# A one-core attention, expert-routing and feed-forward kernel: another order of the last attention steps, of expert 0's weight loads and of two weight splits

## The reference

```python
# 1 attention: batch 2, 8 heads, 768 rows, head size 64
k_sum = k.reshape(B, H, 24, 32, D).max(axis=3);  v_sum = v.reshape(B, H, 24, 32, D).mean(axis=3)
scores_l = q @ k^T / 8, kept where |i - j| < 16;  scores_s = q @ k_sum^T / 8 + log(32)
a = softmax(concat(scores_l, scores_s));  attn = a @ concat(v, v_sum)
# 2 experts: x is attn as 1536 rows of 512; 8 experts of 512 x 1024 x 512
logits = normalized(x) @ normalized(expert_emb).T / tau;  e = argmax(logits)
out[row] = softmax(logits)[e] * (relu(x[row] @ w1[e]) @ w2[e])
# 3 feed-forward, 512 x 2048 x 512
h = relu(out @ w_in);  result = h * h @ w_out
```

## Time and profile before

| | |
|---|---|
| median of 3 runs | 553.11 us (553.05 to 554.74) |
| profiled execution | 553.05 us, span 551.3 us, mean granted PE clock 0.986 |
| busy share of the span | PE 95%, DVE 49%, ACT 43%, POOL 16% |
| attention steps on PE, start to next start | `turn_probs` 0.8 us, `scores` 1.05, `values` 0.85, `fill` 0.6, `turn_pair` 0.8, `ranks` 1.0, `slots` 0.8 |
| steps on DVE | `scale_out` 0.7 us, `row_max` 0.8, `lay_blocks` 2.4, `place` 1.5, `make_hots` 1.6 |
| steps on ACT | `exps` 1.6 us, `regroup_q` 0.7, `move_k` and `move_q` 1.0, `move_prob` 0.45 for one head |

### The profile page before, as it was taken

The page is one execution under the profiler, slowest core; times in us unless marked ns, Lnnn a source line. Parts: engine busy times, 40 slices in busy tenths (PEclk is TensorE's granted clock), DMA queues, the critical chain, the costliest instruction groups (busy, mean ns, idle before and its releaser), DMA issues.

```text
span 551.3 us, 10956 instructions
## 1 busy us (share of the span) xinstructions
PE 523.8 (95%) x4442; PEld 473.1 (86%) x4442; DVE 269.4 (49%) x442; ACT 234.9 (43%) x413; POOL 89.0 (16%) x123
## 2 busy tenths in 40 slices
PE   7498977899999999999999999999999999999997
PEld 6387866789998989989889899899989989989995
DVE  6477877768485864757462232232223223232321
ACT  5478855655676653555531231222223123122221
POOL 5761111212543131260100000000000000000000
PEclk9789999899999999999999999999999999999999
DMA  7956678895679958768110020020001002001001
GB/s 215 257 154 176 186 182 251 251 338 176 251 260 331 312 160 275 263 229 275 64 47 1 0 77 1 1 76 0 0 21 56 0 0 76 0 0 38 2 2 38
DMA packets 62655, 69.50 MB, mean 126 GB/s; under 512 B 22512, under 2 KB 47088, under 8 KB 62232
## 3 DMA queue, kind: packets, MB, share of 16 engines
q1 hardware_dynamic: 59160, 57.36, 32.9%
q0 software_dynamic: 3456, 11.60, 6.2%
HBM read 58.88 MB, written 10.06 MB: 125 GB/s over the span
## 4 chain that ended last, share of the span: by engine, by line
PE 84%; SPq 5%; DVE 4%; DMA 4%; issue 1%; ACT 1%; POOL 0%; DVEq 0%; ACTq 0%; POOLq 0%
PE psum L917 26%; PE psum L918 25%; PE psum L919 25%; DMA k_raw<-in_k 2%; SPq L364 2%; PE psum L911 1%; PE psum L765 1%; PE psum L703 1%; DMA x_rows_sb<-x_rows,gather_tab 1%; SPq L366 1%; PE psum L1021 1%; SPq L363 1%; DVE wb_lo L1627 1%; DVE neg_max L1351 1%; PE psum L830 1%
## 5 line engine op out<-in xcount | busy, mean ns | idle before, releaser
L919 PE MATMUL psum<-x_hi,win_lo 128*128 128x256 f32 x384 | 108.7, 283 | 0.0
L918 PE MATMUL psum<-x_lo,win_hi 128*128 128x256 f32 x384 | 108.7, 283 | 0.0
L917 PE MATMUL psum<-x_hi,win_hi 128*128 128x256 f32 x384 | 108.5, 282 | 0.0
L1725 DVE TENSOR_TENSOR h_sq<-h_relu 128x512 f32<-128x512 f32 x48 | 33.2, 692 | 126.6 <-ACT h_relu L1291 126.6
L1291 ACT ACTIVATE h_relu<-psum 128x512 f32<-128x512 f32 x48 | 28.7, 597 | 127.4 <-PE psum L919 127.4
L917 PE MATMUL psum<-wb_hi,h_hi 128*128 128x512 f32 x208 | 82.4, 396 | 0.0
L919 PE MATMUL psum<-wb_hi,h_lo 128*128 128x512 f32 x208 | 81.1, 390 | 0.0
L918 PE MATMUL psum<-wb_lo,h_hi 128*128 128x512 f32 x208 | 81.1, 390 | 0.0
L918 PEld LDWEIGHTS psum<-x_lo,win_hi 128*128 128x128 f32 x384 | 73.6, 192 | 1.4
L917 PEld LDWEIGHTS psum<-x_hi,win_hi 128*128 128x128 f32 x384 | 73.6, 192 | 1.4
L919 PEld LDWEIGHTS psum<-x_hi,win_lo 128*128 128x128 f32 x384 | 73.6, 192 | 0.0
(11 more groups left out here) (211 smaller groups left out, 878.2 us busy)
## 6 DMA issues: line engine op xcount, KB each, us to landing
w_raw<-in_moe_w SPq DMA_DIRECT2D x56, 512.0 KB, 4.0
win_raw<-in_moe_w_in POOLq DMA_DIRECT2D x8, 512.0 KB, 8.1
w_raw<-in_moe_w_out SPq DMA_DIRECT2D x8, 512.0 KB, 3.6
k_raw<-in_k SPq DMA_DIRECT2D x8, 384.0 KB, 3.6
q_raw<-in_q SPq DMA_DIRECT2D x8, 384.0 KB, 5.5
v_blk<-in_v SPq DMA_DIRECT2D x3, 1024.0 KB, 8.0
v_win<-in_v SPq DMA_DIRECT2D x16, 192.0 KB, 3.9
x_rows<-x_all SPq DMA_DIRECT2D x8, 384.0 KB, 5.4
```

The lines of the kernel that those rows point to most:

```text
L917: pe.matmul(o, l_hi, r_hi, start=start, stop=False)
L918: pe.matmul(o, l_hi, r_lo, start=False, stop=False)
L919: return pe.matmul(o, l_lo, r_hi, start=False, stop=stop)
L1725: dve.tensor_tensor(h_sq[c % 2][:, :], h_relu[c % 2][:, :], h_relu[c % 2][:, :], ALU.mult)\
```

## The change

SP loads all eight parts of block 0 in one go and stores pairs 6 and 7 behind them. POOL loads and splits pieces 6 and 7 of w_in ahead of its loop. On PE, DVE and ACT the steps of the last three attention half-pairs and of batch 0's routing stand in another order. ACT moves more of the turned probabilities and of the turned pairs, in place of DVE, and `values(3, 1, 1)` stands ahead of `turn_rows(0)`.

```diff
@@ SP @@
                 for c in range(2 * PIECES):
-                    if first and c == PIECES:
-                        store_x(PAIRS - 2)
-                        sp.wait_ge(gathered, 32)
                     if not first:
                         sp.wait_ge(w_split[c], b)
...
             load_expert(0, blk_tab0, first=True)
-            store_x(PAIRS - 1)
+            for pr in range(PAIRS - 2, PAIRS):
+                store_x(pr)
@@ POOL @@
             scatter(2, scatter_tab0)
-            with pool.Fori(EARLY, nblk - 2) as b:
-                gather(b + 2, gather_tab)
-                scatter(b, scatter_tab)
             load_win(6)
             load_win(7)
             split_win(6, 3)
             split_win(7, 4)
+            with pool.Fori(EARLY, nblk - 2) as b:
+                gather(b + 2, gather_tab)
+                scatter(b, scatter_tab)
@@ PE @@
             scores(3, 0, 0)
+            pe.wait_ge(logits_moved, 1)
+            turn_probs(2, 1, 0)
+            fill(3, 1, 0)
+            values(2, 1, 0)
             turn_logits(0, 5)
-            fill(3, 1, 0)
+            fill(3, 1, 1)
             pe.wait_ge(logits_read, 1)
-            turn_probs(2, 1, 0)
-            fill(3, 1, 1)
-            pe.wait_ge(consts_made, 2)
-            pe.wait_ge(prob_moved[0], 2 * 5 + 1)
-            pe.wait_ge(prob_moved[1], 2 * 5 + 1)
-            totals(0, 5, at=GT * P)
-            values(2, 1, 0)
-            pe.wait_ge(totals_moved, 1)
-            turn_pair(4)
-            wait_turned(5)
             turn_probs(2, 1, 1)
             scores(3, 0, 1)
             fill(3, 1, 2)
             values(2, 1, 1)
-
+            pe.wait_ge(consts_made, 2)
+            totals(0, 5, at=GT * P)
+            turn_pair(4)
+
+            scores(3, 1, 0)
+            wait_turned(5)
+            pe.wait_ge(totals_moved, 1)
+            turn_probs(3, 0, 0)
             pe.wait_ge(before_made, 1)
             pe.wait_ge(qk_moved_act, 2 * PAIRS)
             ranks(0, 7)
-            scores(3, 1, 0)
-            turn_probs(3, 0, 0)
             values(3, 0, 0)
             turn_pair(5)
             scores(3, 1, 1)
             wait_turned(6)
             turn_probs(3, 0, 1)
+            values(3, 0, 1)
+
+            turn_probs(3, 1, 0)
             slots(0, 7)
-            values(3, 0, 1)
-
-            turn_probs(3, 1, 0)
             values(3, 1, 0)
             turn_pair(6)
             wait_turned(7)
             turn_probs(3, 1, 1)
+            values(3, 1, 1)
...
             turn_rows(0, bank=0)
-            values(3, 1, 1)
             expert_up(0, first=True, behind=weigh_second)
@@ ACT @@
+            move_prob(2, 1, 0)
             exps(2, 1, 1)
             regroup_q(3, 1)
             move_k(3, 1)
-            move_prob(2, 1, 0)
+            move_prob(2, 1, 1)
             exps(3, 0, 0)
+            move_q(3, 1)
             move_pair(4)
-            move_prob(2, 1, 1)
-            move_q(3, 1)
-
-            exps(3, 0, 1)
+
             move_prob(3, 0, 0)
             move_prob(3, 0, 0, hh=1)
-            exps(3, 1, 0)
+            exps(3, 0, 1)
             move_pair(5)
             move_pair(5, half=1)
+            exps(3, 1, 0)
             move_prob(3, 0, 1)
             move_prob(3, 0, 1, hh=1)
 
+            move_prob(3, 1, 0)
+            move_prob(3, 1, 0, hh=1)
             exps(3, 1, 1)
-            move_prob(3, 1, 0)
             move_pair(6)
+            move_pair(6, half=1)
...
             split_hi(wa_hi, wa_hi_made, 0, 0, 16)
             move_prob(3, 1, 1)
+            move_prob(3, 1, 1, hh=1)
             move_x(0, bank=0)
@@ DVE @@
             move_logits(0, 4)
+            move_prob(2, 1, 0)
+            row_max(3, 0, 0)
+            scale_out(2, 1, 0)
             dve.wait_ge(consts_made, 2)
             choose(0, 5)
-            move_prob(2, 1, 0)
-            row_max(3, 0, 0)
             move_kq(3, 1)
-            move_totals(0, 5, at=GT * P)
-            scale_out(2, 1, 0)
-            move_pair(4)
             move_prob(2, 1, 1)
             key_max(3, 1)
             row_max(3, 0, 1)
             scale_out(2, 1, 1)
-
+            move_pair(4)
+            move_totals(0, 5, at=GT * P)
+
+            row_max(3, 1, 0)
             lay_blocks(0, 7)
-            row_max(3, 1, 0)
+            scale_out(3, 0, 0)
             place(0, 7)
+            row_max(3, 1, 1)
             make_hots(0)
-            scale_out(3, 0, 0)
-            row_max(3, 1, 1)
+            scale_out(3, 0, 1)
+
             list_tokens(0, 7)
-            scale_out(3, 0, 1)
-
-            move_prob(3, 1, 0)
             scale_out(3, 1, 0)
-            move_pair(6)
-            move_prob(3, 1, 1)
...
             split_lo(wa_hi, wa_lo, wa_hi_made, 0, 0)
+            scale_out(3, 1, 1)
             move_x(0, bank=0)
-            scale_out(3, 1, 1)
```

More of the change, by code:

```diff
@@ L893, in _ @@
             turn_probs(3, 0, 1)
-            slots(0, 7)
             values(3, 0, 1)
             turn_probs(3, 1, 0)
+            slots(0, 7)
             values(3, 1, 0)
```

## The result

The changed kernel takes 567.59 us (median of 4 runs, 567.53 to 567.76) against 553.92 us before (4 runs, 553.05 to 555.12). The ratio is 1.0246, 95% interval 1.0221 to 1.027. The forecast was 558.2 us in a range of 553.8 to 562.8: the sign was right, the size was not, and the time lies outside the range.

A forecast was written before the change was run, and what follows sets the result against it. PE was taken to bound everything after 103 us, and the routing and gather that release `expert_up(0)` the time before. 553.05 + 1.0 (start) + 3.1 (block 5 wait) + 1.0 (clock) gave 558.2 us, 8-in-10 range 553.8 to 562.8.

The forecast's parts named there:

- part 1: New attention order on PE, DVE and ACT: `gather_tab` and POOL's second gather DMA of block 0 come 0.5 us later.
- part 2: SP's eight weight loads at once: block 0's gather lands beside w2 in 6.5 us, 0.9 us later.
- part 3: `values(3,1,1)` ahead of `turn_rows(0)`: 0.7 us gained at `expert_up(0)`, less 0.3 us for slow clock.
- part 4: POOL's pieces 6 and 7 ahead of its loop: PE waits 3.1 us for `gather(5)`, plus 1.0 us of slow clock.
- the replay: Attention and routing up to `gather_tab`, stepped through in the new order with profiled step times: `gather_tab` at 92.45 us.
- POOL end of 209.0: POOL's two splits ahead of `gather(5)`: done at 208.0 us, plus 1.0 for colliding with DVE's subtractions.
- rival C: Both gathers land in 7.5 us, with a 2 us port collision and 1.2 of clock: 562.7 us, chance 0.20.

The follow-up runs named there:

- the order alone: The kernel before with only the new attention order on PE, DVE and ACT, SP and POOL as before: 555.95 us, ratio 1.0039.
- ACT's order mended: The changed kernel with ACT's `exps(2,1,1)` and `regroup_q(3,1)` put ahead of `move_prob(2,1,0)`: median 566.54 us, four runs from 560.72 to 568.42.
- SP's part alone: The kernel before with only SP's change, no wait for the gather and both pair stores behind the loads: 556.63 us, ratio 1.0058.
- the wait restored: The changed kernel with SP as in the kernel before, waiting for the gather ahead of w2: 564.01 us.
- PE kept busy: The changed kernel with 40 unused transposes ahead of `turn_rows(0)`, while PE waits for the gather: median 562.91 us, runs from 561.06 to 567.25.
- POOL's part alone: The kernel before with only POOL's loads and splits of pieces 6 and 7 moved ahead of its loop: 562.81 us, ratio 1.0187.
- `gather(5)` first: The changed kernel with `gather(5)` taken out of POOL's loop and put ahead of `load_win(6)`: 560.6 us.

## Why the prediction was wrong

The direction and the places were right. The terms of the sum were sized too small, and a half clock inside the attention, which I had put at nothing, took 1.5 us. Forecast against measured, in the profiled executions:

| term | forecast | measured | shown by |
|---|---|---|---|
| part 1, `gather_tab` later | 0.5 us | 2.8 | the order alone; ACT's order mended |
| part 2, landing beside w2 | 0.9 | 2.1 | SP's part alone; the wait restored |
| part 3, `values` and clock | -0.7 + 0.3 | +1.0 together | PE kept busy |
| part 4, wait at block 5 | 3.1 | 6.3 | POOL's part alone; `gather(5)` first |
| part 4, its clock | 1.0 | 2.4 | POOL's part alone (1.4) |
| sum | 5.1 | 14.6 | |

**Part 1.** The step that failed is "`fill` 0.6, `turn_probs` 0.8, `scores` 1.05, `fill` 0.6 give 79.1". I had seen that `move_k` would be 2 us late, and priced it as a later start of steps that run at their usual speed. The wait of 1.78 us that it makes on PE was followed by half clock up to 80.3, and these very steps ended at 81.4, 2.3 us later than in the replay. `move_k` itself was 0.8 us later than replayed (76.84 against 76.0), most of it the hole of 0.70 us in the logits matmuls, which no reading of the trace before could give and which the change does not cause; the other 1.5 us are the half clock. So the replay was right at full clock: with the hole it gives `gather_tab` 24.5 us after the logits matmuls, and the one trace whose clock stays at 1.00 has 24.4. ACT had idled for 4.1 us just ahead of `move_prob(2,1,0)`; moving two steps into that idle time took 2.8 us off the way to `gather_tab`. The DVE term (one more `scale_out` and `row_max`, half given back) was about right: from `ranks` at 86.2 to `gather_tab` at 94.56 it is 8.4 us, and the replay had 8.5.

**Part 2.** I took 6.5 us as a compromise between a row with the same w2 traffic (7.3 to 7.7) and rows with other traffic. The row with the same traffic was the answer, 7.63 us, so the term was 1.2 us too small. The doubt that the page "DMA: Bandwidth & Descriptors" of the Trainium skill raised pulled my value the wrong way; the measurement decides against using its turn-taking rule as protection of a short gather.

**Part 3.** The 0.7 us from moving `values` are there: PE waits for `x_lo`, 0.6 us, in its place, and `expert_up(0)` starts 2.7 us behind the landing in place of 3.4. The clock was under-priced. I counted the half clock behind the landing as if the recovery of the kernel before would be repeated; with the hole of 5.7 us it lasts to 110.9, and 17 matmuls of `expert_up(0)` run at half speed: 1.7 us, where I had 0.3.

**Part 4.** The forecast's POOL end of 209.0 stands at 216.1 - 5.9 = 210.2 in the same frame, so it was 1.2 us early. Two errors partly cancel in it: the load of piece 6 landed in 4.7 us, not 6.0, and the collision added 2.9 us to the splits, not 1.0. The step that failed most is "from its index copy at 191.50 to its second DMA at 193.82, 2.3 us": it became 4.1, as POOL's copy and DMA instructions run slowly beside DVE's subtractions. The landing of 5.5 us was about as forecast here (5.3), but 5.8 to 7.8 in the four other traces that have this wait, so the range needed rival C's 7.5. The page "SBUF — State Buffer" of the Trainium skill, in its account of the shared port pair, says that of a GpSimd operation that reads SBUF and a VectorE operation with two SBUF inputs the one that starts first shuts the other out until it is done. The trace agrees that each holds up the other: DVE's four subtractions were longer by 3.9 us and POOL's steps by 4.7 in all. I had used the rule for the splits and not for the gather behind them. That `scatter(3)` costs 0 held in the changed kernel, where the wait hides it; with the wait gone it costs 0.4 us.

Its clock was under-priced too, 1.0 against 2.4.

Against the checks that the prediction named: `expert_up(0)` started at 107.26, not at 103 to 105; `gather_tab` was written at 94.56, not near 92.5; the last attention transposes came at 97.6, not near 95, and the last `values` at 99.0; PE's hole, its release by the gather and the wait at block 5 were as named. Three slips in the prediction's sums change nothing: 91.1 and 211.4 are 91.0 and 211.3 by their terms, and C's 2.3 at the start is 2.0. Rival C had the right shape (both gathers slow, a collision, a wait of 6.2 us and 1.2 of clock); it is 4.9 us short, 2.3 of it in part 1 and most of the rest the clock. The range was too narrow: even the high ends of all parts at once, 2.9 + 8.4 + 1.5, give 565.9 us. They left out the half clock inside the attention and the hole in the logits, and had at most 1.0 and 1.5 for the clock behind the two gathers, where 1.7 and 2.4 were measured.

## What to carry to other kernels

A step put ahead of an engine's gathers is priced by the whole string behind it, so look for what that engine is due to issue next and when it is wanted: 11 us of work, moved on an engine that was busy for 16% of the span, cost 8.9 us. When a replay of a new order shows a new wait on PE, ask what the steps behind it cost at half clock, and let the range take that in: here a wait of 1.8 us was followed by it in five traces of six. And when a trace has a row with exactly the traffic that the change creates, take that row, not a mean with others.

## What was not expected of the hardware

- The slow clock behind a hole is not in proportion to the hole: behind waits at block 5 of 4.9, 5.7, 6.3, 7.2 and 8.5 us it cost 2.5, 1.4, 2.3, 2.0 and 2.8 us (`turn_rows(5)` to `turn_rows(6)` by PE's timeline, less the 23.3 us of before).
- Nor is it certain. Behind the same wait of 1.8 us for `move_k` the granted clock was 0.50 in five traces and stayed at 1.00 in the sixth, 1.5 us apart at `gather_tab`.
- Beside DVE's subtractions of two SBUF tiles, POOL's index copy takes 1.18 us in place of 0.18 and the issue of an indirect DMA 1.75 in place of 1.0. Whether PE would gain from keeping them apart was not tried.
- The second 128-row gather of block 0 lands in 4.7 to 6.1 us with 2 MB of weights queued and in 7.3 to 7.6 with 4 MB. The time of the kernel before spreads by 0.8% over 18 runs, while in the traces blocks 1 to 6 repeat to 0.1 us where no gather or scatter is late.
